# Ten slots for the free tokens in the routing's counts, and an attention loop with update and keys moved and the state scaled on ScalarE

## The reference

```python
# attention, for each position t
state = alpha[:, :, t, :, None] * state + np.einsum('bhd,bhe->bhde', k[:, :, t], v[:, :, t])
y[:, :, t] = np.einsum('bhd,bhde->bhe', q[:, :, t], state)

# routing: pairs (token, expert) from the highest logit down
logits = x @ w_gate
for idx in np.argsort(-logits.flatten()):
    tok, e = idx // E, idx % E
    if assigned[tok] >= 0 or counts[e] >= cap:
        continue
    assigned[tok] = e
    counts[e] += 1
for e in range(E):
    mask = assigned == e
    out[mask] = np.maximum(x[mask] @ w1[e], 0.0) @ w2[e]

# gated layer
g = x @ w_gate2
out = ((g * sigmoid(g)) * (x @ w_val)) @ w_out
```

## Time and profile before

| | before |
|---|---|
| median of 3 runs | 874.03 us (872.48 to 876.46) |
| the profiled execution | 874.86 us, its span 873.0 us |
| PE busy | 835.8 us, 96% |
| DVE busy | 558.7 us, 64% |
| ACT busy | 280.0 us, 32% |
| POOL busy | 276.8 us, 32% |
| mean granted TensorE clock | 0.984 of full speed |

### The profile page before, as it was taken

The page is one execution under the profiler, slowest core; times in us unless marked ns, Lnnn a source line. Parts: engine busy times, 40 slices in busy tenths (PEclk is TensorE's granted clock), DMA queues, the critical chain, the costliest instruction groups (busy, mean ns, idle before and its releaser), DMA issues.

```text
span 873.0 us, 17172 instructions
## 1 busy us (share of the span) xinstructions
PE 835.8 (96%) x6425; PEld 792.0 (91%) x6425; DVE 558.7 (64%) x1065; ACT 280.0 (32%) x505; POOL 276.8 (32%) x263
## 2 busy tenths in 40 slices
PE   8899995699989999999999999999999999999995
PEld 5788884499989999999999999999999999999995
DVE  8999986757865665566556755675567556742332
ACT  1344443322323333333333333333333323333221
POOL 3222210179736041604150515051506050604001
PEclk9999997799999999999999999999999999999998
DMA  8899952500320041004100410031013001300000
GB/s 328 292 355 357 319 201 90 172 1 1 110 63 27 0 126 45 27 0 134 37 27 6 134 36 22 20 126 34 18 37 116 27 18 48 105 28 19 1 1 30
DMA packets 26001, 77.25 MB, mean 88 GB/s; under 512 B 3824, under 2 KB 10480, under 8 KB 23152
## 3 DMA queue, kind: packets, MB, share of 16 engines
q1 hardware_dynamic: 19440, 62.67, 20.8%
q0 software_dynamic: 3072, 9.44, 3.2%
q10 hardware_dynamic: 3456, 4.72, 1.5%
HBM read 67.38 MB, written 9.44 MB: 88 GB/s over the span
## 4 chain that ended last, share of the span: by engine, by line
PE 74%; DVE 6%; issue 2%; ACT 1%; DMA 0%; POOL 0%; POOLq 0%; DVEq 0%; ACTq 0%
PE ps_up L1634 44%; PE ps_acc L1634 27%; PE ps_turn_again L891 1%; DVE quick_at_row L829 1%; DVE u_low L1602 1%; DVE act_out L1599 1%; ACT u_high L1538 1%; PE ps_turn L1640 1%; PE ps_turn_again L911 0%; DVE act_out L1595 0%; PE ps_turn_again L771 0%; DVE quick_at_row L741 0%; DMA x_tok<-x_rows,slot_token 0%; PE ps_up L1640 0%; POOL x_tok L1493 0%
## 5 line engine op out<-in xcount | busy, mean ns | idle before, releaser
L1438 POOL TENSOR_TENSOR w_low<-w_raw,w_high 128x384 fp32r<-128x384 f32 x120 | 150.4, 1280 | 229.8 <-ACT w_high L1519 228.8
L1634 PE MATMUL ps_up<-z_high,gated_high 128*128 128x384 f32 x576 | 199.2, 346 | 0.2 <-DVE z_low L1590 0.2
L1634 PE MATMUL ps_up<-z_high,gated_low 128*128 128x384 f32 x576 | 195.5, 339 | 0.0
L1634 PE MATMUL ps_up<-z_low,gated_high 128*128 128x384 f32 x576 | 193.0, 335 | 0.0
L1538 ACT CAST u_high<-act_out 128x384 fp32r<-128x384 f32 x96 | 49.2, 513 | 190.9 <-DVE act_out L1599 190.9
L1634 PEld LDWEIGHTS ps_up<-z_high,gated_high 128*128 128x128 f32 x576 | 108.4, 188 | 0.6 <-issue 0.5
L1634 PEld LDWEIGHTS ps_up<-z_high,gated_low 128*128 128x128 f32 x576 | 108.5, 188 | 0.0
L1634 PEld LDWEIGHTS ps_up<-z_low,gated_high 128*128 128x128 f32 x576 | 108.3, 188 | 0.0
L1634 PE MATMUL ps_acc<-gated_high,u_high 128*128 128x384 f32 x288 | 97.6, 339 | 3.0 <-DVE u_low L1602 3.0
L1634 PE MATMUL ps_acc<-gated_high,u_low 128*128 128x384 f32 x288 | 97.1, 337 | 0.0
L1634 PE MATMUL ps_acc<-gated_low,u_high 128*128 128x384 f32 x288 | 97.0, 337 | 0.0
(11 more groups left out here) (179 smaller groups left out, 1467.6 us busy)
## 6 DMA issues: line engine op xcount, KB each, us to landing
w_raw<-in_experts SPq DMA_DIRECT2D x64, 384.0 KB, 3.0
qka_in<-in_qka SPq DMA_DIRECT2D x22, 1026.0 KB, 7.8
gated_raw<-in_gated SPq DMA_DIRECT2D x12, 576.0 KB, 6.8
v_in<-in_v SPq DMA_DIRECT2D x24, 192.0 KB, 7.0
x_rows<-y_rows ACTq DMA_DIRECT2D x24, 192.0 KB, 5.4
qka_in<-in_qka SPq DMA_DIRECT2D x2, 512.0 KB, 6.4
qka_in<-in_qka SPq DMA_DIRECT2D x1, 514.0 KB, 6.5
out<-o_tok,to_rows POOLq DMA_INDIRECT x24, 2.6
```

The costliest lines, as they stand in the source:

```text
L1438: part = pool.tensor_tensor(w.low[:, m % RING, cols], w.raw[:, m % RING, cols], w.high[:, m % RING, cols].bitcast(F32), ALU.subtract)
L1634: mm = pe.matmul(acc, lhs[a], rhs[b], start=(first and i == 0), stop=(last and i == 2))
```

## The change

Three things change.

In the phases 1 to 7 two new steps come first. They number the free tokens of each partition by a running sum, and copy their best logit and their expert's number into ten slots (`slot_best`, `slot_choice`). The comparisons and counts of the three rounds then go over 10 slots instead of 24 tokens. A round takes two steps instead of three, so that a phase has 15 steps instead of 16. The matmuls of `ps_token` come in one step instead of two.

In the attention PE does the update between own and carried, and the keys ahead of the scores. The last update (unit 20) is left out.

The multiplication of the state by the chunk's end decay moves from DVE to ACT, as four instructions, with a fifth that reads the end decay itself into `ends`. The next scan into the same `decay` buffer waits for that fifth (`ends_scaled`), and DVE's addition waits for carried (`y_cols_ready`).

```diff
-                    dve.wait_ge(state_ready, u - 3)
+                    dve.wait_ge(ends_scaled, u - 3)
                     dve.wait_ge(q_ready, u - 3)
...
                 dve.wait_ge(update_ready, u + 1)
+                dve.wait_ge(y_cols_ready, u + 1)
+                if u >= B:
+
+                    dve.wait_ge(state_ready, u - 3)
                 dve.tensor_tensor(state[b][:, :, :].rearrange("p a e -> p (a e)"), ps_state[:, 0:PAIRS * D],
                                   state[b][:, :, :].rearrange("p a e -> p (a e)"), ALU.add).then_inc(state_added, 1)
-                dve.wait_ge(state_added, u + 1)
-                end = decay[b][:, :, P:SEG].broadcast_to([P, PAIRS, D])
-                dve.scalar_tensor_tensor(out=state[b][:], in0=state[b][:], scalar=1.0 / DECAY_UNIT, in1=end,
-                                         op0=ALU.mult, op1=ALU.mult).then_inc(state_ready, 1)
...
+            def end_scale(i, j):
+                u, b, c = unit(i, j)
+                act.wait_ge(decay_ready, u + 1)
+                act.mul(ends[j % 2][:], decay[b][:, :, P], 1.0 / DECAY_UNIT).then_inc(ends_scaled, 1)
+
+            def state_scale(i, j):
+                u, b, c = unit(i, j)
+                act.wait_ge(ends_scaled, u + 1)
+                act.wait_ge(state_added, u + 1)
+                for a in range(PAIRS):
+                    scaled = act.mul(state[b][:, a, :], state[b][:, a, :], ends[j % 2][:, a:a + 1])
+                scaled.then_inc(state_ready, 1)
+
+            def step(i, j, first=False, ahead=True, split_after={1: 0, 3: 1}, scaled=True, to_scale=True):
+                if scaled and not first:
+                    state_scale(i, j - 1)
                 y_cols_copy(i, j)
...
                 if ahead:
                     k_copy(i, j + 2)
+                if to_scale:
+                    end_scale(i, j)
                 if j in split_after:
                     w.split_gated_high(act, i - 1, split_after[j])
...
-                outputs(i, j, first_chunk)
-                if ends:
-                    pe.wait_ge(state_ready, UNITS - B + 1)
-                    quick.turn_ends(pe)
+                own_outputs(i, j, first_chunk)
+                if not first_chunk:
+
+                    pe.wait_ge(state_ready, u - 3)
                 if updated:
                     if not first:
 
-                        pe.wait_ge(state_ready, u)
+                        pe.wait_ge(state_added, u)
                     update(i, j)
+                if not first_chunk:
+                    carried_outputs(i, j)
...
                     gate_and_turn(i, j - 1)
+                if keys:
+                    keys_of(i, j + 2)
                 if ahead:
-                    front(i, j + 2, keys=keys)
+                    scores_of(i, j + 2)
...
-                step(CH - 1, j, ahead=(j < 2), keys=False, updated=(j == 0), ends=(j == B - 1))
+                step(CH - 1, j, ahead=(j < 2), keys=False, updated=False, ends=(j == B - 1))
...
-FINE_TILES = (slice(0, 15), slice(15, TILES))
+SLOTS = 10
...
-    TAKE = 3 * FINE_ROUNDS
+    SEARCH = 2
+    TAKE = SEARCH + 2 * FINE_ROUNDS
     STEPS_A_PHASE = TAKE + 7
...
+        n, finding = divmod(s - self.SEARCH, 2)
+        by_slot = [P, SLOTS, TILES]
+        if s == 0:
+
+            link(dve.tensor_scalar(self.free, self.best[:], -0.1 * BIG, None, ALU.is_gt))
+            link(dve.tensor_tensor_scan(self.place, self.free, self.zeros[:], 0.0, ALU.add, ALU.add))
+            link(dve.tensor_tensor(self.place, self.place, self.free, ALU.mult))
+            link(dve.tensor_tensor(self.held, self.place.unsqueeze(1).broadcast_to(by_slot),
+                                   self.numbers[:, 1:SLOTS + 1].unsqueeze(2).broadcast_to(by_slot), ALU.is_equal))
+            link(dve.tensor_tensor(self.numbered, self.choice[:],
+                                   self.numbers[:, 1:E + 1].unsqueeze(1).broadcast_to(te), ALU.mult))
+            link(dve.tensor_reduce(self.number, self.numbered, AX_X, ALU.add))
+        if s == 1:
+            for of, into in ((self.best[:, :], self.slot_best), (self.number, self.slot_number)):
+                link(dve.tensor_tensor(self.held_part, self.held, of.unsqueeze(1).broadcast_to(by_slot), ALU.mult))
+                link(dve.tensor_reduce(into[:], self.held_part, AX_X, ALU.add))
+            se = [P, SLOTS, E]
+            link(dve.tensor_tensor(self.slot_choice[:], self.slot_number[:, :].unsqueeze(2).broadcast_to(se),
+                                   self.numbers[:, 1:E + 1].unsqueeze(1).broadcast_to(se), ALU.is_equal))
+        if self.SEARCH < s <= take and not finding:
+            self.raise_base(dve, self.rounds_before(p) + n, self.fine_cuts[:, n - 1, 0:1])
+        if self.SEARCH <= s < take and not finding:
+            self.compare(dve, self.slot_best[:, :], slice(0, SLOTS), self.fine_cuts[:, n, :])
+        if self.SEARCH <= s < take and finding:
             self.find_full(dve, self.rounds_before(p) + n + 1, FINE_CUTS - 1)
...
+            pe.wait_ge(self.over_cut_ready, ROUNDS + self.rounds_before(p) + n + 1)
+            for j in range(SLOTS):
+                mm = pe.matmul(self.ps_count, self.at_row[:, j, :], self.slot_choice[:, j, :],
+                               start=(j == 0), stop=(j == SLOTS - 1))
             mm.then_inc(self.cuts_counted, 1)
```

More of the change, by code:

```diff
@@ L66, in attention @@
         state = [sb(f"state{b}", [P, PAIRS, D]) for b in range(B)]
+        ends = [sb(f"ends{r}", [P, PAIRS]) for r in range(2)]
         y_rows = [sb(f"y_rows{r}", [P, DM]) for r in range(2)]
@@ L327, in store @@
                 act.dma_start(x_rows[b, c], y_rows[b % 2][:]).then_inc(stored[b % 2], 16)
-            def step(i, j, first=False, ahead=True, split_after={1: 0, 3: 1}):
+            def end_scale(i, j):
[12 more added lines that the diff above has]
+                    state_scale(i, j - 1)
                 y_cols_copy(i, j)
@@ L393, in outputs, with carried_outputs @@
                                        scores[j % 2][:, h, :], start=(a == 0), stop=(first_chunk and a == PAIRS - 1))
-                if not first_chunk:
-                    for a in range(PAIRS):
-                        for g in range(2):
-                            rows = slice(HALF * g, HALF * g + D)
-                            mm = pe.matmul(ps_y_cols[rows, a * P:(a + 1) * P], state[b][rows, a, :],
-                                           q_dec[b][rows, a, :], start=False, stop=(a == PAIRS - 1))
+                if first_chunk:
+                    mm.then_inc(y_cols_ready, 1)
+            def carried_outputs(i, j):
+                u, b, c = unit(i, j)
+                for a in range(PAIRS):
+                    for g in range(2):
+                        rows = slice(HALF * g, HALF * g + D)
+                        mm = pe.matmul(ps_y_cols[rows, a * P:(a + 1) * P], state[b][rows, a, :],
+                                       q_dec[b][rows, a, :], start=False, stop=(a == PAIRS - 1))
                 mm.then_inc(y_cols_ready, 1)
@@ L906, in tensor_step @@
                       stop=True).then_inc(self.mine_ranked, 1)
-        if s in (take + 3, take + 4):
-            i = s - take - 3
-            pe.wait_ge(self.at_row_ready, 2 * p + i + 1)
-            for t in range(i * TILES // 2, (i + 1) * TILES // 2):
-                mm = pe.matmul(self.ps_token, self.at_row[:, t, :],
-                               self.token_parts[:, t, :, :].rearrange("p a c -> p (a c)"),
-                               start=(t == 0), stop=(t == TILES - 1))
+        if s == take + 4:
+            for i in range(2):
+                pe.wait_ge(self.at_row_ready, 2 * p + i + 1)
+                for t in range(i * TILES // 2, (i + 1) * TILES // 2):
+                    mm = pe.matmul(self.ps_token, self.at_row[:, t, :],
+                                   self.token_parts[:, t, :, :].rearrange("p a c -> p (a c)"),
+                                   start=(t == 0), stop=(t == TILES - 1))
             mm.then_inc(self.tokens_ready, 1)
```

71 lines of the change are left out of this document (38 added, 33 removed).

## The result

The changed kernel takes 899.19 us (median of 4 runs, 898.64 to 900.92) against 874.92 us before (4 runs, 872.48 to 876.46). The ratio is 1.0288, 95% interval 1.026 to 1.0317. The prediction said 864, with 0.07 for slower.

What follows compares the result with a forecast made beforehand. TensorE was taken as the bound in the attention's loop and the experts. Counting -7.0, first chunk -1.5, group order -1.0, last update -0.6 and expert 0 at 0 sum to -10.1: 863.9, said as 864 us, range 859 to 870.

Steps and rivals of the forecast that it cites:

- the part on the pack: Steps 0 and 1 of a phase on DVE: eleven small instructions come in, later comparisons shrink and stay hidden; cost nothing.
- Rival D: The pack stalls every phase behind POOL's splittings: 1.8 us a phase, up to 880 us in all; chance 0.05.
- The clock: Start of the experts: an earlier start shifts where a TensorE half-speed stretch falls, worth 1.7 us either way.
- Counting over ten slots: Routing phases: 10 count matmuls instead of 24 and one group less save 1.17 us a phase, 7.0 us over six.
- The pack at nothing: Routing phases: the packing instructions on DVE stay covered by TensorE's work, costing 0; done at about 356.
- Expert 0: Routing beside POOL's long run of splits: delays and gains cancel, 0 us, bounds -4.8 and +3.
- rival B: Expert 0 gets worse as routing moves deeper into POOL's run: +3 to +5 us, 867 to 869; chance 0.15.
- The last update: Attention's last chunk: the update of unit 20 goes from TensorE's path, saving 0.60 us.
- The first chunk: Attention's first chunk: DVE loses the state's scaling, so TensorE waits less; 1.5 us saved, bounds 0.8 and 1.6.
- The order of the groups: Attention's loop: the new matmul order takes 5.31 us a unit, 0.06 less; 1.0 us over 16 units, bounds +1.6 and -2.6.
- The scaling: Attention on ACT: five more instructions a unit, 0.6 to 1.0 us, fit in the unit; no gain or loss in the loop.
- rival A: Attention's loop: waits for the ends make a ring that sets the pace, 5.8 us a unit, about 872; chance 0.12.

Runs made afterwards that it cites:

- experiment 11: The changed kernel with two extra one-input reductions on VectorE ahead of the first comparison of a phase; 905.8 us.
- experiment 5: The changed kernel with one empty step ahead of the search, so a phase's first comparison is issued inside GpSimd's run of splittings; 867.19 us.
- 13: The kernel of experiment 5 with a one-element GpSimd memset, without any wait, between the last indirect store and the splittings; 870.83 us.
- experiment 3: The changed kernel, with GpSimd in experts 1 to 6 waiting for the phase's first comparison before its run of splittings; 858.74 us, ratio 0.9823.
- experiment 1: The kernel before with only the attention's edits, routing as before; 868.03 us, ratio 0.9929.
- experiment 9: The kernel of experiment 1 with the scaling of the state back on DVE; 870.0 us, ratio 0.9936.
- experiment 15: The changed kernel with a one-element GpSimd memset and a wait for its semaphore between the last indirect store and the splittings; 859.84 us, ratio 0.9835.
- experiment 7: The kernel before with an unused tensor of 240 bytes a partition where the changed kernel puts its slots; 874.6 us, ratio 1.0005.

## Why the prediction was wrong

**The step that failed** is in the part on the pack: "Later a comparison covers 990 elements, about 1.24 us instead of 2.9, and stays hidden." 1.24 us is right, hidden is not: the first comparison of a phase took 7.53 us, of which TensorE waited 4.28, and a stretch at half clock followed. I looked at where the pack's own instructions lie against POOL's run (it begins "after the pack") and not at the first instruction behind the pack. Before, the first comparison of a phase stood at 351.42, six microseconds ahead of the run; the pack pushed it to 0.7 us ahead. My own numbers had it there: with the pack done at 356 and an `h_low` of 0.56 us behind it, the comparison begins some 0.9 us ahead of 357.41. "After the pack" was true and of no use. The move of an instruction along a queue was costed only by what the queue itself waits for, not by what another engine does at the new place.

**Rival D** of the prediction had the right engines at the wrong instructions, and its price was too low. I took one splitting as the longest wait, as the 1.12 against 0.36 us of the earlier trace rows suggested; it is the whole run. By D a phase loses 1.8 us, by the runs 6.6. The Trainium skill, SBUF — State Buffer, section on who interferes with whom, lets the loser wait until the other engine's instruction has finished; experiment 11 agrees on which operations are concerned, but where the page speaks of one instruction the changed kernel measured a wait for all six, and experiments 5 and 13 for the rest of the six.

**The clock** was in the prediction only as something that the start of the experts shifts, ±1.7 us. That came too: the first 18 products of the experts took 4.95 us before, at half clock, and 3.38 in experiment 3, at full clock. But a new wait of 4.3 us brought a new half-clock stretch each time, about 2.3 us; one of 1.3 us in experiment 5 brought none. Between them it was not the same each time: the wait of 2.28 us that ended at 248.58 in the kernel before brought no such stretch, and the same wait in experiment 1, 2.30 us long, brought one of 3.4 us.

**Counting over ten slots** (-7.0): right. A count takes 0.26 us to the next product (376.93 to 377.19), and without the hold the period is the 85.2 us that was forecast. That is partly chance: in the chain of work of one period, counts give 1.05 us, 18 products of `ps_up` take 3.12 us instead of 3.16, which gives 0.5, and new short waits around `z_low` take some 0.3 back.

**The pack at nothing:** the pack itself was as forecast, 348.71 to 353.16.

**Expert 0** (0, bounds -4.8 and +3): without the hold the stretch to expert 1's gated layer is 2.5 us shorter, but that is not expert 0's doing: 1.6 are the clock of its first products, and the counts of two phases, 2.2, lie in it. From the gated layer of expert 0 to that of expert 1, the distance that the prediction named as the sign, experiment 3 takes 91.5 us (189.80 to 281.31) against 91.25, with one phase's 1.2 already off. So expert 0 itself lost some 1.4, between the forecast and rival B. The prediction also laid all of the 4.85 us of the earlier trace rows on POOL's run of 33 us. But 2.28 of them are TensorE's wait that ended at 248.58, for a `u_low` that began 22 us after that run was over: it is the hold behind an indirect transfer.

**The attention:** forecast -3.1 in all, measured some -6 to the experts. The last update gives its 0.6 (4.78 to 4.18 us for that unit), but only with the scaling on ACT: in experiment 9 that unit takes 4.79 us, as TensorE then waits 0.53 us for masked scores. The first chunk gives 0.55 in experiment 1 and not 1.5, since TensorE still waits four times for masked scores, 2.4 us. The order of the groups gives 16 x 0.30 = 4.8 us and not 1.0. (The terms as written, 0.88, 0.70, 1.00, 1.07 and 1.68, add up to 5.33 and not 5.31, so 0.6 and not 1.0.) Own to update took 0.91 us, about as forecast. Update to carried took 0.55 and not 0.70: the price of a change of rows was not there. Of "The others keep their lengths" only carried held: turn went from 1.07 to 0.97, keys and scores together from 1.68 to 1.62. The scaling is worth nothing in the loop (experiment 9), as said, and rival A did not come: DVE waited 3.8 us in all for the ends.

**The sum without the hold.** Experiment 3's span is 16.0 us below before (857.0 against 873.0), where the sum had 10.1. Of the difference the attention has 2.9 and the clock at the start of the experts 1.6. So the other terms were near by and large, and what turned a gain into a loss is the one step above.

## What to carry to other kernels

When an edit shifts an instruction, look up in the trace what every other engine does at its new place, and read the old trace for an instruction that took several times its usual length: 3.87 us for a 0.56 us operation was there to be found. Where GpSimd goes from indirect transfers straight to a run of elementwise work, a one-element `memset` and a wait for its semaphore in between cost it some 0.3 us (347.97 to 348.26 in experiment 15) and spare VectorE the run. A wait of TensorE of 4.3 us cost 6.6 here, and filling it with idle products gave back only the clock's part.

## What was unexpected of the hardware

The hold to a run's end behind an indirect transfer, 4.85 us against 1.24 at the same place behind a rest of 0.17 us; its cause inside the engine was not shown. That it is taken early: a comparison issued 0.69 us ahead of the first splitting's start lost. That the time of a TensorE group hangs on the group behind it by 0.05 to 0.11 us in most pairs (update to turn 0.60, update to carried 0.55; own to carried 1.02, own to update 0.91). And one thing stays open: the 18 products of `ps_up` take 3.16 us in the kernel before and with the attention's half alone, 3.12 us in the kernels with the slots, and experiment 7 only ruled out the 240 bytes.
